# Router logits of four token tiles in four column tiles of TensorE, the scores matmuls placed earlier, and the first weight loads queued behind the stores

## What is computed

```python
# attention: B=4, H=8, S=768, D=48
for t in range(S):
    cur = einsum('bhd,bhe->bhde', u * k[t], v[t])
    y[t] = einsum('bhd,bhde->bhe', r[t], state + cur)
    state = w * state + einsum('bhd,bhe->bhde', k[t], v[t])
x = y as (3072 tokens, 384)
# first layer: only tokens with x @ w_skip > 0; N=3072, D=384, E=8, F=1024
logits = x @ w_gate;  e = argmax(logits);  gate = softmax(logits)[e]
out = x + gate * (relu(x @ w1[e]) @ w2[e])       # other tokens: out = x
# second layer: all tokens
logits = x @ w_gate2; e = argmax(logits);  gate = softmax(logits)[e]
out = gate * (relu(x @ w1b[e]) @ w2b[e])
```

## Time and profile before

| | us |
|---|---|
| median of three runs | 688.5 |
| the runs | 685.23, 688.5, 690.48 |
| the profiled execution | 690.23 |
| its span in the trace | 688.5 |

### The profile page before, as it was taken

The page is one execution under the profiler, slowest core; times in us unless marked ns, Lnnn a source line. Parts: engine busy times, 40 slices in busy tenths (PEclk is TensorE's granted clock), DMA queues, the critical chain, the costliest instruction groups (busy, mean ns, idle before and its releaser), DMA issues. The chain is left out here.

```text
span 688.5 us, 17341 instructions
## 1 busy us (share of the span) xinstructions
PE 624.1 (91%) x6081; PEld 603.2 (88%) x6082; DVE 401.4 (58%) x772; ACT 253.8 (37%) x647; POOL 322.8 (47%) x391
## 2 busy tenths in 40 slices
PE   4999999957599999899929997999999999999994
PEld 3789988847589999899929997899999999998994
DVE  5877777727736777877700035648375683836432
ACT  2123233214035555456602210635255462525221
POOL 4876677705156666566620003536254453535321
PEclk9999999977889999999965569999999999999997
DMA  7476666951137666566353600255252624011100
GB/s 150 107 161 151 137 139 153 282 207 61 49 108 219 213 204 203 158 206 196 99 138 110 229 0 16 85 179 174 85 163 97 228 105 147 22 46 38 46 22 22
DMA packets 113728, 88.78 MB, mean 129 GB/s; under 512 B 80475, under 2 KB 104724, under 8 KB 113680
## 3 DMA queue, kind: packets, MB, share of 16 engines
q1 hardware_dynamic: 106304, 74.16, 35.7%
q0 software_dynamic: 7376, 14.03, 7.8%
HBM read 79.06 MB, written 13.57 MB: 135 GB/s over the span
## 5 line engine op out<-in xcount | busy, mean ns | idle before, releaser
L735 DVE TENSOR_TENSOR w_lo<-w_raw,w_hi 128x384 fp32r<-128x384 f32 (+1 forms) x158 | 130.9, 854 | 1.7 <-issue 1.3
L973 PE MATMUL e_ps_y<-w_hi,hidden 128*128 128x384 f32 x344 | 120.0, 349 | 0.0
L975 PE MATMUL e_ps_y<-w_hi,hidden 128*128 128x384 f32 x344 | 115.6, 336 | 0.0
L974 PE MATMUL e_ps_y<-w_lo,hidden 128*128 128x384 f32 x344 | 115.1, 335 | 0.0
L730 ACT CAST w_hi<-w_raw 128x384 fp32r<-128x384 f32 (+1 forms) x224 | 114.1, 555 | 1.0 <-PEq L42 0.3
L735 POOL TENSOR_TENSOR w_lo<-w_raw,w_hi 128x512 fp32r<-128x512 f32 (+1 forms) x66 | 87.9, 1354 | 31.9 <-ACT w_hi L730 31.6
L1056 ACT CAST e_x_hi<-e_ps_x 128x384 fp32r<-128x384 f32 x47 | 22.5, 478 | 134.8 <-PE e_ps_x L959 125.0
L889 POOL DMA_INDIRECT rows<-x_rows,e_ent_in x47 | 51.0, 1084 | 40.0 <-POOL e_ent_in L885 40.0
L973 PE MATMUL e_ps_h<-e_x_hi,w_hi 128*128 128x256 f32 x228 | 64.8, 284 | 5.2 <-DVE e_x_lo L1120 3.1
L973 PE MATMUL e_ps_ht<-e_x_hi,w_hi 128*128 128x256 f32 x228 | 64.7, 284 | 2.9 <-DVE hidden L1160 2.9
L974 PEld LDWEIGHTS e_ps_y<-w_lo,hidden 128*128 128x128 f32 x344 | 64.9, 189 | 0.0
(11 more groups left out here) (156 smaller groups left out, 1356.8 us busy)
## 6 DMA issues: line engine op xcount, KB each, us to landing
w_raw<-in_moe_w_dram SPq DMA_DIRECT2D x32, 1536.0 KB
r_in<-in_r_dram SPq DMA_DIRECT2D x24, 192.0 KB, 2.7
k_in<-in_k_dram SPq DMA_DIRECT2D x24, 192.0 KB, 3.4
v_in<-in_v_dram SPq DMA_DIRECT2D x24, 192.0 KB, 3.6
x_rows<-rows SPq DMA_DIRECT2D x24, 192.0 KB, 3.1
w_lo<-x_rows SPq DMA_DIRECT2D x4, 768.0 KB, 5.3
m_placing<-x_rows SPq DMA_DIRECT2D x2, 768.0 KB, 7.2
rows<-x_rows,e_ent_in POOLq DMA_INDIRECT x47
```

Source lines behind the costliest of these rows:

```text
L735: eng.tensor_tensor(self._of(self.lo1[par], self.lo2[par], n), self._of(self.raw1[par], self.raw2[par], n), self._of(self.hi1[par], self.h ...
L973: pe.matmul(o, s_hi, m_hi, start=(k == 0), stop=False)
L974: pe.matmul(o, s_hi, m_lo, start=False, stop=False)
L975: return pe.matmul(o, s_lo, m_hi, start=False, stop=(k == last))
```

## The change

In attention the logits of four tiles are formed together, once in four steps. `xT` now holds four transposed tiles. `logitsT` (in the step with sub = 1) takes `w_g`, padded with zeros to 32 columns, as weights and the transposed tiles as moving operand, 128 columns each; tile b writes partitions 32b to 32b+31 of `ps_x`, a column tile of its own: 12 matmuls. ScalarE copies the result (`logitsT_out`) to `lT`, one transpose brings it back (`logits`, in the step with sub = 2), and ScalarE copies the logits of all four tiles out (`logits_out`). The scores (L369) now stand before the state's part (L363). The last group's logits are formed after the last step.

On SP's queue the two loads of expert 0 come after the stores of the rows 20 and 21; those of expert 1 are issued at the start of the first route, those of expert 2 by `moe`. In the first route no remainders are formed; VectorE forms all 14 in `moe`: six before it takes the first gathered rows, eight after the second `x_low`.

In the second route the same scheme replaces `logits_of`; the copies of the transposed tiles are split, tiles 0 and 2 of a group to ScalarE and 1 and 3 to VectorE. VectorE clears `w_g` at the start, and SP waits for that too.

```diff
@@ attention
-        xT = sb("xT", [P, CH, P])
+        xT = sb("xT", [P, B, CH, P])
+        lT = sb("lT", [P, P])
@@ sync
-            sp.wait_ge(dve_zeroed, 1)
+            sp.wait_ge(dve_zeroed, 2)
...
-            for par in range(2):
-                for matrix in range(2):
-                    W.load(sp, matrix, 0, par, par)
             for sub in range(STEPS - B, STEPS):
+                if sub == STEPS - 2:
+                    for matrix in range(2):
+                        W.load(sp, matrix, 0, 0, 0)
                 store(0, sub)
@@ scalar: step
                 decay(c, sub)
-                if not (isinstance(i, int) and i < 2):
-                    logits_out(i - 2)
+                if sub == 1 and not (isinstance(c, int) and c == 0):
+                    logitsT_out(c - 1)
+                if sub == 2 and not (isinstance(c, int) and c == 0):
+                    logits_out(c - 1)
                 if not (isinstance(i, int) and i == 0):
-                    x_out(i - 1)
+                    x_out(c, sub - 1) if sub else x_out(c - 1, B - 1)
@@ tensor
             def turn_x(c, sub):
                 wait(pe, row_done, i + 1)
-                wait(pe, l_out, i)
+                wait(pe, xT_out, i)
+                if sub % B == 0:
+                    wait(pe, lT_out, c + sub // B)
+                if sub % B == 1:
+                    wait(pe, l_out, c + sub // B)
...
-            def logits(i):
-                wait(pe, xT_out, i + 1)
+            def logitsT(c):
+                pe.wait_ge(gates_loaded, 48)
+                wait(pe, xT_out, B * c + B)
                 for m in range(CH):
-                    ins = pe.matmul(ps_x[:, HD:HD + G], xT[:, m, :], w_g[:, m, :], start=(m == 0), stop=(m == CH - 1))
-                ins.then_inc(l_ready, 1)
+                    for b in range(B):
+                        ins = pe.matmul(ps_x[GP * b:GP * b + GP, HD:HD + P], w_g[:, m, :], xT[:, b, m, :], start=(m == 0), stop=(m == CH - 1), skip_group_check=True)
+                ins.then_inc(lT_ready, 1)
+            def logits(c):
+                wait(pe, lT_out, c + 1)
+                if not (isinstance(c, int) and c == STEPS // B - 1):
+                    wait(pe, xT_out, B * c + B + 1)
+                pe.transpose(ps_x[:, HD:HD + P], lT[:], ident[:]).then_inc(l_ready, 1)
@@ tensor: step (the matmuls of ps_y moved behind those of ps_a)
+                if sub == 2 and not (isinstance(c, int) and c == 0):
+                    logits(c - 1)
...
                 ins.then_inc(scored, 1)
-                    logits(i - 2)
+                if sub == 1 and not (isinstance(c, int) and c == 0):
+                    logitsT(c - 1)
+                wait(pe, row_done, i - 1)
+                wait(pe, state_done, i - 1)
+                for p in range(NP):
+                    for t in (slice(0, P // 2), slice(P // 2, P)):
+                        pe.matmul(ps_y[n][t, 2 * p:2 * p + 2, :].rearrange("p j d -> p (j d)"), r_sc[n][:, p, t], state[b][:, p, :], start=(p == 0), stop=False, skip_group_check=True)
@@ route: sync
-            for k in range(2):
-                W.wait_split(sp, k, W.E // 2 * m, 0)
-                W.load(sp, k, m, 2, 0)
+            if not TURN:
+                for k in range(2):
+                    W.load(sp, k, 0, 1, 1)
+            if TURN:
+                for k in range(2):
+                    W.wait_split(sp, k, W.E // 2, 0)
+                    W.load(sp, k, 1, 2, 0)
@@ route: gpsimd
-            if not TURN:
-                for n in range(W.N1):
-                    W.lo(pool, 0, 0, n)
@@ route: tensor
+            def logitsT(g):
+                for n in range(2):
+                    pe.wait_ge(xT_out[n], GRP // 2 * (g + 1))
+                if g:
+                    pe.wait_ge(l_out, g)
                 for c in range(CH):
+                    for b in range(GRP):
+                        ins = pe.matmul(ps_l[GW * b:GW * b + GW, 0, :], w_g[:, c, :], xT[:, b, c, :], start=(c == 0), stop=(c == CH - 1), skip_group_check=True)
+                ins.then_inc(lT_ready, 1)
+            def logits_of(g):
+                pe.wait_ge(lT_out, g + 1)
+                pe.transpose(ps_l[:, 1, :], lT[:], ident[:]).then_inc(l_ready, 1)
...
-                for i in range(TILES + 2):
+                for i in range(GRP):
+                    turn_x(i)
+                for g in range(TILES // GRP):
+                    logitsT(g)
+                    if g + 1 < TILES // GRP:
+                        for i in range(GRP * (g + 1), GRP * (g + 2)):
+                            turn_x(i)
+                    logits_of(g)
@@ route: scalar (vector: x_out(dve, g, 1) for each g)
                 for g in range(TILES // GRP):
+                    x_out(act, g, 0)
+                    logitsT_out(g)
+                    logits_out(g)
@@ route: vector, at the end
-            if not TURN:
-                for n in range(W.N1, W.N):
-                    W.lo(dve, 0, 0, n)
@@ moe: sync
+            if m == 0:
+                follow(0, 0, 0, 2)
@@ moe: vector
+            if m == 0:
+                for n in range(W.N1):
+                    W.lo(dve, 0, 0, n)
             dve.wait_ge(gathered, 16)
             dve.tensor_copy(x_row[:], x_in[:]).then_inc(x_taken, 1)
             x_low(0, 0)
...
             x_low(1, 1)
+            if m == 0:
+                for n in range(W.N1, W.N):
+                    W.lo(dve, 0, 0, n)
             take(2)
```

More of the change, by code:

```diff
@@ L39, in attention @@
     TABLE_STEPS = 20
-    G = w_g.shape[2]
+    G = lg.shape[2]
+    GP = w_g.shape[2]
     CH = HD // P
@@ L198, in _, with x_out, logitsT_out, logits_out @@
             act.wait_ge(tables, 8)
-            def x_out(i):
+            def x_out(c, sub):
+                i = 4 * c + sub
                 wait(act, x_turned, i + 1)
[L203 to L208, removed]
+                act.copy(xT[:, sub % B, :, :], ps_x[:, 0:HD].rearrange("p (c t) -> p c t", c=CH)).then_inc(xT_out, 1)
+            def logitsT_out(c):
+                wait(act, lT_ready, c + 1)
+                act.copy(lT[:], ps_x[:, HD:HD + P]).then_inc(lT_out, 1)
+            def logits_out(c):
+                wait(act, l_ready, c + 1)
+                act.copy(lg[:, bass.ds(B * c, B), :], ps_x[:, HD:HD + P].rearrange("p (b g) -> p b g", b=B)[:, :, 0:G]).then_inc(l_out, 1)
             def decay(c, sub):
@@ L239, in _ @@
             dve.memset(w_col[:], 1.0).then_inc(dve_zeroed, 1)
+            dve.memset(w_g[:], 0.0).then_inc(dve_zeroed, 1)
             dve.wait_ge(small, 48)
@@ L355, in step @@
                     turn_rk(c, sub + 1)
[L357 to L363, removed]
+                c, sub = c + sub // B, sub % B
+                if sub == 2 and not (isinstance(c, int) and c == 0):
+                    logits(c - 1)
+                if isinstance(i, int):
+                    pe.wait_ge(scaled, 2 * i + 2)
+                    wait(pe, masked, 2 * i)
                 for p in range(NP):
@@ L393, in _ @@
             run_steps(pe, step)
-            logits(STEPS - 2)
             turn_x(0, STEPS - 1)
-            logits(STEPS - 1)
+            logitsT(STEPS // B - 1)
+            logits(STEPS // B - 1)
 def route(nc, m, W, x_rows, ident, w_g, lg, hot, table, starts, order, stored):
@@ L419, in route @@
     GRP = 512 // P
+    GW = w_g.shape[2]
     TURN = m == 1
@@ L466, in route @@
         if TURN:
-            turned_x = [sb(f"turned_x{n}", [P, CH * P]) for n in range(4)]
+            xT = sb("xT", [P, GRP, CH, P])
+            lT = sb("lT", [P, P])
             spare = W.lo2[1][:].bitcast(F32)
@@ L471, in route @@
                     placing[:, 0:GRP * CH * P].rearrange("p (b d) -> p b d", b=GRP)]
-        ps_l = [ps(f"ps_l{n}", [P, GRP, E]) for n in range(2)]
+        ps_l = ps("ps_l", [P, 2, P])
         ps_places = ps("ps_places", [P, 512])
@@ L481, in route @@
         x_loaded = [sem(f"x_loaded{g}") for g in range(TILES // GRP)] if TURN else []
-        x_turned = sem("x_turned"); xT_out = sem("xT_out"); l_ready = sem("l_ready"); l_out = sem("l_out")
+        x_turned = sem("x_turned"); xT_out = [sem(f"xT_out{n}") for n in range(2)]; lT_ready = sem("lT_ready"); lT_out = sem("lT_out"); l_ready = sem("l_ready"); l_out = sem("l_out")
         made = sem("consts_made")
@@ L496, in load_rows, with x_out @@
                     eng.dma_start(x_in[g % len(x_in)], x_rows.rearrange("(b c p) d -> c p b d", b=GRP, p=P)[g]).then_inc(x_loaded[g], 16)
+        def x_out(eng, g, n):
+            for b in range(n, GRP, 2):
+                if g:
+                    eng.wait_ge(lT_ready, g)
+                eng.wait_ge(x_turned, GRP * g + b + 1)
+                copy = eng.copy if n == 0 else eng.tensor_copy
+                copy(xT[:, b, :, :].rearrange("p c t -> p (c t)"), ps_xT[b][:, 0:CH * P]).then_inc(xT_out[n], 1)
         def rows_hot(eng, n):
@@ L551, in turn_x @@
                 ins.then_inc(x_turned, 1)
[L553 to L558, removed]
```

(24 more changed lines are left out.)

24 lines of the change are left out of this document (8 added, 16 removed).

## The result

The changed kernel takes 650.25 us (median of 4 runs, 642.76 to 655.57) against 686.87 of the kernel before beside it: ratio 0.944, interval 0.932 to 0.957. Two more sets of runs, on other occasions, gave ratios of 0.935 (0.929 to 0.940) and 0.946 (0.939 to 0.953). The ratios and their intervals leave out the executions that were slow as a whole (one of these four). The profiled execution was the fastest of the four: 642.76, span 641.1, 47.4 less than the span before, while the medians fell by 36.6.

What follows compares the result with a forecast made beforehand. TensorE was taken to bound attention's loop and the experts, and to be busy throughout route 2 at clock 0.51. Terms summed to -44.7: 690.2 profiled became 645.5, 644 as median (1.7 lower); range 635 to 660.

Steps and rivals of the forecast that it cites:

- Attention's loop, -10: Attention's loop: 21 steps fall from 5.40 to 4.68 us, plus five times 1.0 for logits, 113.4 to 103.3.
- VectorE's circle: Attention's loop: the chain through VectorE's masks, 1.35 + 1.39 + 1.94 = 4.68 us, against TensorE's 4.63.
- Attention's end, -10.8: End of attention: wait for a store gone -6.9, tail -3.2, last step without L341 -0.7; bounds -13, -7.
- The tail: End of attention, from 149.99 to 158.57: 8.6 us before, 5.4 forecast, so -3.2.
- The term of -3.8: End of route 1: eight remainders go, -3.8 us.
- Start of `moe`, +0.3: Before the first experts' matmuls: remainders reappear on VectorE, +0.3 us; upper bound if they hold POOL's gathers.
- the sentence on expert 2's loads: In `moe`: the load starts some 20 us later, is wanted an expert after that, and stays hidden behind the experts.
- Route 2, -17: Route 2's logits: groups of four tiles, 4.15 us at full clock, 6.2 at half; clock rises after the first group.
- rival (a): Route 2 stays at half clock or swings: -6.5 instead of -17 and no -2, total 656; chance 0.25.
- (b): `logitsT`: the four column tiles do not overlap, 2.9 instead of 0.9 us, 12 times, total 668; chance 0.06.
- (c): Attention's loop: VectorE or POOL sets the step at 5.1 instead of 4.68, total 653; chance 0.1.
- (d): Slower than before: new waits drop the clock to half in attention's loop, all 24 steps give 733; chance 0.01.

Runs made afterwards that it cites:

- x123: Changed kernel with expert 2's loads after the second gather, route 2 reordered, nine instead of six idle turns before route 1's placing matmuls: 639.2 us.
- x2: Changed kernel with SP issuing expert 2's loads only after the second gather of rows has landed: 641.9 us, ratio to before 0.934.
- x4: Kernel of x123 with four instead of two turns of idle transposes ahead of route 2's first rows: 637.9 us, ratio to before 0.933.
- after_again: The changed kernel unaltered, run once more for a second trace: 642.3 us against 684.57 of before.
- b_only: Kernel before with only the weight loads behind the stores and expert 0's remainders moved to the experts' block: 674.9 us against 684.57.
- c_only: Kernel before with only the second route's part of the change and the padded `w_g`: 664.1 us against 684.57.
- after_third: The changed kernel unaltered, run once more as the measure for two others: 647.5 us, ratio to before 0.946.

## Why the prediction was right

The forecast was 644 within 635 to 660, the measured medians 650, 642 and 648. The forecast sum was -44.7; the span of the profiled execution fell by 47.4, the medians by 36.6, 42.3 and 38.4. So the total held, and the mechanisms of the three parts with it. That it held this well is in part luck: terms were off in both directions (attention 2.3 and route 2 5.2 more than forecast; route 1's end 0.9, the start of `moe` 1.9, the rest after it 0.5 and 2.1 less), and the profiled execution is one that had full clock in all of route 2's logits.

**Attention's loop, -10: too small.** The step was to be 4.68, VectorE's circle, and came at 4.60: TensorE has no gap and its own work sets the step. A step with `logitsT` took 0.68 more, where 1.0 was taken for it and the transpose back. Over the 21 steps the shorter step makes 1.7 and the five cheaper `logitsT` 1.6, and the loop fell by 13.4. From the start of the last scores times v (149.99 to 128.91, -21.1) the wait of 6.86 goes off, and 14.2 are left for 10.0 and the last step's 0.7. The claim that the order of the scores carries this gain (a step of 5.3 without it) was tested and held: 5.29.

**Attention's end, -10.8: too large (-9.5).** The wait went as said. The tail was to fall from 8.6 to 5.4 (the terms written down add up to 5.3) and took 6.7 (128.91 to 135.61): 0.53 in front of the last pass of L416, and the clock, at half when route 1 began. With the first `moe`'s start these are the places where the forecast took the short passes of the full clock for granted.

**Route 1.** L633's successor took 0.36, the scan came 1.7 earlier. The term of -3.8 held (the time from the table to the block's end fell by 4.4), but the placing matmuls took 8.72 instead of 7.20, at a clock of 0.55 from 150 to 155: +1.5 that no step had. `x123` took it back with longer idle turns.

**Start of `moe`, +0.3 (bounds -1.5, +2.5): +2.2, and 1.9 more in the first expert.** The upper end was put down to POOL's gathers being held by the remainders. They are held: the first issue took 1.56 instead of 1.23, the copy behind it 0.72 instead of 0.19. That is the smaller part. The step that failed is the sentence on expert 2's loads, which asked only whether the load comes in time, not what it stands in front of: it filled the DMA engines (share 0.95 from 165 to 170) just when the second gather was due. `x2` shows it: 13.2 to 9.9, which is 1.1 less than before the change. The 1.9 in the first expert come from passes of 0.41 at the half clock. The rule on VectorE and POOL in the Trainium skill, "SBUF — State Buffer", "Who interferes with whom", agrees with the rows: 0.36 against 1.38 in route 1, 3.78 against 0.69 in the second `moe`. But the 3.78 outlast three operations of POOL in a row, where the prediction reckoned with one piece at a time.

**Route 2, -17: -22.2.** Mechanism right, two sizes off. From the start of the transpose back to the next `logitsT` it takes 1.31 (343.19 to 344.50), where 1.75 were added up, so a group takes 3.47 and not 4.15: 3.4 of the 5.2 missed. The rest is the clock, up from the first group on. Executions with part of the stage at half took 22.7 to 25.3 with the same groups: rival (a) describes what eight of the ten profiles do for 3 to 12 us, and none for the whole stage; its 656 never came as a median. The Trainium skill, "TensorE: Matmul & The Clock Gate", Part 4, holds that transposes don't count as activity for the clock. By that rule `x4`'s 32 idle transposes would have had no effect; the granted clock was 0.50 at their start and 1.00 before their end, with nothing else on TensorE.

**The rivals.** (b) fell: 0.79 and not 2.9. (c) fell: no gap on TensorE at 4.60. (d) fell: clock 1.00 all through the loop.

## What to carry to other kernels

An operation of few columns with large weights on TensorE can cost twice: its own time, and, where it fills much of a stage as in route 2, the clock of everything around it (attention, with 0.77 us of it in a step of 5.40, kept 1.00). Making the small operand the weights, four tiles at a time in column tiles, mended both here. Taking work out of a loop's bound pays only if the next circle is shortened too: here a step of 5.40 fell to 5.29 without the new order, and to 4.60 with it. And when a large load is moved to a later place, look at which small transfer is due behind it: here a gather landed 3.3 us late and took back that much of what the move gave.

## What was not expected of the hardware

- Four column tiles of 32 columns, float32, 128 columns moving: 24 passes in 0.79 us at full clock, 0.033 each; 1.45 at half (336.64 to 338.09 in `after_again`).
- The old logits, weights of 128 columns and 8 columns moving, lost the full clock although TensorE was busy for 10.1 of 11 us (`b_only`); the new groups gained it (`c_only`) and kept it while TensorE was busy for only 14.7 of 21 us (the kernel after). Busy time as the profile counts it doesn't tell which.
- The same kernel ran route 2's logits wholly at 1.00 (the kernel after) or with 10 us at 0.50 (`after_again`, `after_third`), which is worth 4 us. TensorE waited 0.8 us for the rows behind its idle transposes in the first case and 2.2 in the others; that the wait decides it is likely, not shown.
- A VectorE operation with two inputs from SBUF took 3.78 us instead of 0.69 while POOL issued a gather and had two such operations of its own at work.
